# Loading q and k of a small-head attention in runs of tokens, and sorting heads on TensorE

## What is computed

```python
for c in range(nc):                       # chunks of 32 tokens
    l_start = max(0, c_start - 16); r_end = min(S, c_end + 8)
    k_full = concat([mem_k, k[:, :, l_start:r_end]], axis=2)
    v_full = concat([mem_v, v[:, :, l_start:r_end]], axis=2)
    scores = scale * q_c @ k_full.T
    a = exp(scores - max); a = a / (sum(a) + 1e-9)
    out[:, :, c_start:c_end] = a @ v_full
x = attn_out as [3072, 512]
x = elu(x @ w_in) @ w_out                 # layer 1
h = relu(x @ w_in2); out = (s * h * h + b) @ w_out2   # layer 2
```

## Time and profile before

| | us |
|---|---|
| median of 3 runs | 1153.65 (1152.37 to 1153.94) |
| the profiled execution | 1152.69 |
| its span on the core | 1151.0 |
| head, to the first feed-forward step | about 99 |
| woven stage, about | 110 to 450 |

### The profile page before, as it was taken

The page is one execution under the profiler, slowest core; times in us unless marked ns, Lnnn a source line. Parts: engine busy times, 40 slices in busy tenths (PEclk is TensorE's granted clock), DMA queues, the critical chain, the costliest instruction groups (busy, mean ns, idle before and its releaser), DMA issues.

```text
span 1151.0 us, 18156 instructions
## 1 busy us (share of the span) xinstructions
PE 1100.9 (96%) x5787; PEld 876.8 (76%) x5787; DVE 843.8 (73%) x1258; ACT 767.7 (67%) x1806; POOL 392.1 (34%) x427
## 2 busy tenths in 40 slices
PE   7989988989899999989999999999999999999998
PEld 4767666767677777768788787887888888888886
DVE  4895787368957956896887968868848569576485
ACT  4886786577657757756758667667666366674564
POOL 5788789751231432234276113653000000000000
PEclk8998999989999999999999999999999999999999
DMA  9998999999799889859899789998697666776664
GB/s 210 258 272 260 348 321 354 347 286 327 212 269 249 259 244 272 274 184 329 306 357 343 242 260 376 298 351 273 194 275 233 189 198 186 216 220 190 195 189 158
DMA packets 204055, 302.81 MB, mean 263 GB/s; under 512 B 112824, under 2 KB 121016, under 8 KB 203960
## 3 DMA queue, kind: packets, MB, share of 16 engines
q1 hardware_dynamic: 203960, 301.65, 84.9%
HBM read 226.10 MB, written 75.50 MB: 262 GB/s over the span
## 4 chain that ended last, share of the span: by engine, by line
PE 68%; DMA 7%; ACT 6%; POOL 6%; DVE 5%; issue 4%; SPq 4%; ACTq 0%; POOLq 0%; DVEq 0%
PE ps L1003 33%; PE ps L988 30%; DMA w_scratch<-w_new 4%; POOL w_new L786 2%; ACT ps L1083 2%; DMA w_ring<-w_scratch 1%; POOL att L786 1%; ACT elu L1169 1%; PE ps L900 1%; DVE g_lo L1464 1%; SPq L592 1%; PE ps L925 1%; ACT elu L1174 1%; PE ps L952 1%; DVE X L1381 1%
## 5 line engine op out<-in xcount | busy, mean ns | idle before, releaser
L988 PE MATMUL ps<-xc_hi,w_ring 128*128 128x512 f32 x1344 | 435.4, 397 | 6.1 <-DVE X L1433 3.1
L1003 PE MATMUL ps<-g_hi,w_ring 128*128 128x512 f32 x1344 | 421.7, 395 | 15.9 <-issue 7.6
L1003 PEld LDWEIGHTS ps<-g_hi,w_ring 128*128 128x128 f32 x1344 | 249.6, 189 | 75.4 <-issue 14.9
L988 PEld LDWEIGHTS ps<-xc_hi,w_ring 128*128 128x128 f32 x1344 | 253.9, 189 | 64.1 <-issue 3.2
L988 PE MATMUL ps<-xc_lo,w_ring 128*128 128x512 f32 x672 | 263.2, 392 | 0.0
L1003 PE MATMUL ps<-g_lo,w_ring 128*128 128x512 f32 x672 | 263.2, 392 | 0.0
L786 POOL TENSOR_TENSOR w_new<-w_raw,w_new 128x256 fp32r<-128x256 f32 x179 | 165.8, 932 | 226.7 <-ACT w_new L1222 223.8
L1464 DVE TENSOR_TENSOR g_lo<-X,g_hi 128x512 fp32r<-128x512 f32 x240 | 176.9, 741 | 26.1 <-ACT g_hi L1208 25.4
L1208 ACT ACTIVATE g_hi<-X 128x512 fp32r<-128x512 f32 x240 | 148.8, 627 | 62.2 <-PE ps L1003 59.8
L1381 DVE TENSOR_TENSOR X<-s,ps 128x512 f32<-128x512 f32 x144 | 96.1, 682 | 104.6 <-ACT s L1145 77.1
L1003 PEld LDWEIGHTS ps<-g_lo,w_ring 128*128 128x128 f32 x672 | 126.9, 189 | 27.0
(11 more groups left out here) (117 smaller groups left out, 1339.2 us busy)
## 6 DMA issues: line engine op xcount, KB each, us to landing
w_ring<-w_scratch SPq DMA_DIRECT2D x336, 512.0 KB, 4.4
w_scratch<-w_new SPq DMA_DIRECT2D x179, 256.0 KB, 5.3
w_scratch<-att SPq DMA_DIRECT2D x45, 256.0 KB, 5.3
w_raw<-in_moe_w_in SPq DMA_DIRECT2D x16, 512.0 KB, 6.2
w_raw<-in_moe_w_out SPq DMA_DIRECT2D x16, 512.0 KB, 6.2
x_scratch<-y SPq DMA_DIRECT2D x12, 512.0 KB, 6.2
att<-x_scratch SPq DMA_DIRECT2D x12, 512.0 KB, 6.3
out<-elu SPq DMA_DIRECT2D x24, 256.0 KB, 4.4
```

The costliest lines, as they stand in the source:

```text
L988: last = nc.tensor.matmul(bank_of(st.pi, st.i), w[:, a, cols], x[:, st.pi, kk, :], start=(st.pi in (P1, P5, P4) and kk == 0 and n == 0), s ...
L1003: last = nc.tensor.matmul(bank_of(st.pi, d), w[:, a, cols], x[:, k % RING, :], start=(st.pi in (P1, P5) + (P4,) * (1 - st.gr) and st.i == ...
```

## The change

- q is loaded in runs of 6 tokens: a partition holds one head and 6 tokens (6 x 64 floats, 1536 bytes in one piece), 16 runs of 8 heads make 128 partitions.
- k and the memory keys are loaded in runs of 8 tokens (2048 bytes), 15 runs of 8 heads for a full unit and one run for the memory.
- A partition now holds one head of several tokens, so a plain transpose no longer gives what is wanted. For each of the 8 (k) or 6 (q) places in the run and each of two halves, PE multiplies: weights are the 128 x 64 block of data, the moving operand is 64 columns of the identity, sorted by head (`heads_of`, a new tile that POOL copies from `ident`, behind a wait on it). That is 16 products for k in place of 4 transposes, and 12 for q.
- Heads are paired otherwise: the halves now hold heads 0 to 3 and 4 to 7. The product with v reads its probabilities accordingly; what it writes and in what order is as before.
- DVE's copy to `kT` and ACT's copy to `qT` put the tokens in order: they read PSUM with a step of 64 floats and write in one piece.
- PE waits for `ident_done` 4 in place of 3.

```diff
+RUNS = KEYS // MEM
+Q_RUN, K_RUN = QU // RUNS, MEM
...
+        heads_of = sb("heads_of", [128, 2, PAIRS, RUNS])
...
         def q_of(n):
-            return qk_of(n)[0:QU, 0:512]
+            return qk_of(n)[:, 0:Q_RUN * D]
...
+            def runs(src, b, lo, hi, r):
+                return src[bass.ds(b, 1), :, lo:hi, :].rearrange("b h (g r) d -> g (b h) (r d)", r=r)
...
-                sp.dma_start(heads(q_of(n)), rows(q, b, blk * QU, blk * QU + QU)).then_inc(done, 16)
-                sp.dma_start(heads(k_of(n)[lo - first:hi - first]), rows(k, b, lo, hi)).then_inc(done, 16)
-                sp.dma_start(heads(k_of(n)[CTX:KEYS]), rows(mem_k, b, 0, MEM)).then_inc(done, 16)
+                sp.dma_start(q_of(n), runs(q, b, blk * QU, blk * QU + QU, Q_RUN)).then_inc(done, 16)
+                sp.dma_start(k_of(n)[lo - first:hi - first], runs(k, b, lo, hi, K_RUN)).then_inc(done, 16)
+                sp.dma_start(k_of(n)[CTX:KEYS], runs(mem_k, b, 0, MEM, K_RUN)).then_inc(done, 16)
...
+            pool.wait_ge(ident_done, 3)
+            nc.gpsimd.tensor_copy(heads_of[:, :, :, :], ident[:, :].rearrange("p (g e j) -> p e j g", e=2, j=PAIRS))\
+                .then_inc(ident_done, 1)
...
-                for j in range(PAIRS):
-                    last = nc.tensor.transpose(kT_bank(n)[:, j, :], k_of(n)[:, j * 128:(j + 1) * 128], ident[:, :])
+                for r in range(K_RUN):
+                    for e in range(2):
+                        last = nc.tensor.matmul(kT_bank(n)[64 * e:64 * e + 64, r], k_of(n)[:, r * D:(r + 1) * D],
+                                                heads_of[:, e], start=True, stop=True)
...
-                for j in range(PAIRS):
-                    last = nc.tensor.transpose(qT_bank(n)[:, j, :], q_of(n)[:, j * 128:(j + 1) * 128],
-                                               ident[0:QU, 0:QU])
+                for r in range(Q_RUN):
+                    for e in range(2):
+                        last = nc.tensor.matmul(qT_bank(n)[64 * e:64 * e + 64, r], q_of(n)[:, r * D:(r + 1) * D],
+                                                heads_of[:, e], start=True, stop=True)
...
-            pe.wait_ge(ident_done, 3)
+            pe.wait_ge(ident_done, 4)
...
-                nc.scalar.activation(qT[slot_of(n)][:, :, :], qT_bank(n), ACT.Copy, scale=SCALE).then_inc(qT_sb, 1)
+                nc.scalar.activation(qT[slot_of(n)].rearrange("p j (g r) -> p j g r", r=Q_RUN),
+                                     qT_bank(n).rearrange("p r j g -> p j g r"), ACT.Copy, scale=SCALE).then_inc(qT_sb, 1)
...
-                nc.vector.tensor_copy(kT[slot_of(n)][:, :, :], kT_bank(n)).then_inc(kT_sb, 1)
+                nc.vector.tensor_copy(kT[slot_of(n)].rearrange("p j (g r) -> p j g r", r=K_RUN),
+                                      kT_bank(n).rearrange("p r j g -> p j g r")).then_inc(kT_sb, 1)
```

More of the change, by code:

```diff
@@ L393, in kT_bank @@
         def kT_bank(n):
-            return pairs(7, 128, KEYS)
+            return bank[7][:, :].rearrange("p (r j g) -> p r j g", r=K_RUN, j=PAIRS)
         def qT_bank(n):
-            return pairs(7 if n < HEAD else 6, 128, QU)
+            return bank[7 if n < HEAD else 6][:, 0:PAIRS * QU].rearrange("p (r j g) -> p r j g", r=Q_RUN, j=PAIRS)
         def X_bank(n):
@@ L921, in p_times_v @@
                 pe.wait_ge(PT_sb[1], n + 1)
[L922 to L926, removed]
+                for h in range(H):
+                    half = slice(64 * (h % 2), 64 * (h % 2) + 64)
+                    last = nc.tensor.matmul(X_bank(n)[half, h // 2, :], v_of(n)[:, h * D:(h + 1) * D],
+                                            PT[slot_of(n)][:, h // PAIRS, h % PAIRS, :], start=True, stop=True)
                 last.then_inc(pv_done, 1)
```

## The result

| | before | after |
|---|---|---|
| median, us | 1153.8 (1152.37 to 1155.89, 4 runs) | 1163.22 (1163.12 to 1164.16, 4 runs) |
| the profiled execution | 1152.69 | 1164.16 |
| its span | 1151.0 | 1162.4 |

The changed kernel is slower: ratio 1.0082, interval 1.0066 to 1.0099, +9.4 us. The forecast was +4.7 us, in a range that holds the result. The sign and PE's prices were right, the size was half of the measured one, and the start of the program went the other way.

The account below looks back on a forecast made before the run. PE was taken to bound the kernel, in a loop with DVE in the head and by its steps when woven; head -2, last seven woven units +7.7, first eight 0 made +5.7, taken at +5: 1158.5 us, range 1145 to 1175.

Parts of the forecast that it names:

- PE's price for k and q: PE's added work in a head turn: k +0.44 us and q +0.42 us.
- the columns' pace: PE's new products: columns set the time, 0.055 us for a pair of records of 64 columns.
- rival C: PE's products: weights set the pace, 0.082 us a pair, +18 us on the forecast, 1177 us; chance 0.11.
- The turn: Head: PE sets the turn, 4.42 + 0.44 + 0.42 = 5.28 us, 0.72 more than 4.56.
- change of form: PE: switch to products that write half the partitions, 0.09 us; moved ahead of k, one more for q.
- the disturbances of the head: 13 head turns: 7.9 us of late k, waiting for ACT and slow clock, all taken as gone; +0.7 net.
- The start: Program start to unit 3's scores: second k lands at 8.6 us, not 10.8; -2.7 us if the clock stays up.
- The woven stage: Woven units: PE +1.1 us each; +7.7 in the last seven, 0 in the first eight, bounds -9 and +9.
- The last discount: Sum of all terms: +5.7 us taken at +5, since small waits late in the woven stage shrink too.
- Rival A: First eight woven units: PE's addition hidden, -9 remains; head -5; total -6, 1148 us; chance 0.25.
- rival B: PE pays everywhere: first eight woven units +8.8, head clock falls once (+3); 1170 us; chance with Rival D 0.19.
- Rival D: DMA: longer pieces don't help, start and k waits stay; +5 us on the forecast; chance 0.19 with rival B.

Follow-up runs that it names:

- e2: Kernel before with only PE's 28 products, loads as before (attention not computed rightly): 1167.43 us, ratio 1.0105.
- e5: Changed kernel without the two idle products in each head turn from the fourth on: 1157.79 us, ratio 1.0039 to the kernel before.
- e4: Changed kernel with units 0 and 1 loaded and transposed in the old form: 1164.81 us, ratio 1.0073 to the kernel before.
- e6: Changed kernel with the first raw weights (512 KB) asked for after unit 1's loads: 1162.57 us, ratio 1.0077 to the kernel before.
- e1: Kernel before with only the loads in runs, PE's transposes as before (attention not computed rightly): 1142.85 us, ratio 0.9884.
- e3: Kernel before with k and the memory in runs and sorted in every unit, q as before: 1153.01 us, ratio 0.9987.
- e11: e8 with q also in runs in the first eight woven units: 1147.69 us, ratio 0.995 to the kernel before.
- e9: Kernel before with only units 0 and 1 in the new form, loads and products: 1153.67 us, ratio 0.9998.
- e10: e7 without the two idle products in each head turn from the fourth on, raw weights in their old place: 1145.89 us, ratio 0.993 to the kernel before.
- e8: e7 without the two idle products a turn and with the first raw weights asked for after unit 1's loads: 1144.07 us, ratio 0.9921 to the kernel before.
- e7: Kernel before with k in runs in units 2 to 24, everything else as before: 1146.59 us, ratio 0.9942.

## Why the prediction was half of what came

**PE's price for k and q: right.** k was to take 0.9 to 1.0 us and q 0.75 to 0.85; they take 0.98 and 0.85. A pair of records is (0.98 - 0.09) / 16 = 0.056 us, the 0.055 of the columns' pace, not the 0.082 of rival C; k's row of 32 records is 1.15 us long and q's of 24 is 0.92, which is 0.058 for each of the four pairs more. By the rule for weight loads on the Trainium skill's page TensorE: Matmul & The Clock Gate, LDWEIGHTS, an estimate for k's 32 loads of 64 columns is 1.7 us; the row has 0.98, so the rule doesn't hold here.

**The turn: 5.40, forecast 5.28.** I charged one more change of form and had the one behind k disappear. By the rows, q grew by 0.46 and k by 0.45, the probabilities ahead of k by 0.09 (0.66 to 0.75), and the product with v behind it gave back only 0.04 (0.81 to 0.77). I had counted k's change of form as moved and not added. The missing 0.12 in the 12 turns that have a k is the 1.4 us of the second line of the table.

**That the disturbances of the head go: right, the reason only in part.** PE's wait for ACT at 85.77 is gone, and the clock's fall with it. e2 has neither without any relief for DMA, so PE's longer turns are enough. This rests on one execution of each kernel. POOL's waits for its buffers were to fall below 10 us; they fell from 20.1 to 13.2.

**The start: the step that failed.** Forecast -2.7, measured +2.0 in the profiled execution. The step was "k of the second unit lands two units' saving earlier, 8.6 in place of 10.8". It took 354 GB/s, the rate of the seventh slice, for transfers issued in the first microseconds. The rows have 180 GB/s from 2 to 6 us and about 240 up to 14, and no more bytes in all than before. With the raw weights in their old place no trace with loads in runs has the second k before 11.10. I also costed SP's issue at nothing, and it takes 0.1 to 0.45 us more for each q and k. The 4.7 us split so: the second k is 3.2 us later than forecast (12.24, 9.0), and from there to the scores of unit 3 it takes 16.8 in place of 15.4, because the clock was still at its lower level for 3.4 us, which costs 1.7. Two signs named for a wrong forecast, the wait for k and the clock's early fall, both came. Of the 4.7 only 2.5 are in e5's trace of the same code too (26.86, forecast 24.4); the other 2.2 are the difference of two executions.

The step had a second fault: it added the start's gain to the total as it stood. e4 and e6 reach unit 3 2.4 and 1.7 us sooner than the changed kernel, and their medians don't show it. So the runs show that the -2.7 did not come, and that not all of it would have lasted; how much of the missed 4.7 us of the median is the start's stays open.

**The woven stage: right in sum, with a better account now.** +6.8 us against +6.6 in the last six intervals. An undisturbed unit costs 1.25 us more (21.95 and 20.70), above my 1.1; one of the six hides half of it. For the first eight I took 0 between bounds of -9 and +9; it was +0.05. That it came so close is luck: two intervals gave 3.4 us and the other six cost 3.4. e1 and e2 show two opposite parts, -4.8 and +3.4, and e3 and e11 that the balance is not the same for k and q. Rival A (all of PE's work hidden there, the saving of DMA taken) would have needed -9, rival B +8.8; neither came.

**The last discount.** I took +5 for a sum of +5.7, "since small waits late in the woven stage shrink too". The last six intervals show no such thing. It was a number without a row.

**Rival D** (longer pieces don't help) holds for the first 10 us and is refuted later: e1 is 10.8 us faster than the kernel before.

**Left open.** Why the DMA engines are only 0.69 busy from 2 to 6 us with long pieces isn't settled. The form of the first two units does it, since e9, with all later units short, has 0.71, as e6 has with other bytes behind the loads. The longer issue on SP is a candidate, but no run took the issue's length away by itself. Nor is it settled which wait in the first eight woven intervals takes what e4 and e6 had gained at the start.

## What to carry to other kernels

Longer pieces that need sorting afterwards trade DMA time for time of the engine that sorts, so price the trade stage by stage and operand by operand, and put it only where DMA's relief ends a wait: here k in 23 of 32 units gave 0.6%, and k and q everywhere cost 0.8%. A gain in one stage counts only as far as the next stage lets it through. A transfer rate read in a full stretch of the program isn't that of its first transfers; take the start's gain from rows of the start, or take none. When real work is added to an engine that was kept busy with idle products, try it without them, and look at the clock in the stages behind.

## What the hardware showed that was not expected

- An issue on SP takes longer for a load in runs: for the second unit's k 0.90 us with 120 pieces of 2048 bytes and 0.54 with 960 of 256.
- Reading PSUM with a step of 64 floats and writing in one piece costs DVE 0.69 us for 128 x 512, and 0.68 without the step.
- With the first two units in runs the DMA engines were busy with a share of 0.69 to 0.73 from 2 to 6 us and moved 168 to 182 GB/s (five traces); with short pieces the share was 1.00 to 1.10 and the rate 187 to 208 GB/s (seven traces). The engines had time left, and still less was moved.
- Two float32 products of 64 columns, one into each half of the partitions, take 0.056 to 0.058 us together, with a new load of weights for each (k's 0.98 us less 0.09 for 16 pairs; k's row 0.23 us longer than q's for four pairs more).
- Without the two idle products in a turn the granted clock was 0.66 in 95 to 100 us (e10) and 0.55 in 90 to 95 us (e8), where e7, with them, has 1.00; e5, also without them but with longer turns, has 1.00 in 90 to 120 us.
